# Linear attention and two expert stages on one core: a unit's outputs stand ahead of the next unit's state sum on TensorE

## The reference, cut to what matters

```python
gamma = 1.0 - 2.0 ** (-5.0 - np.arange(H))
for t in range(S):                      # B, H, S, D = 4, 8, 768, 64
    state = gamma * state + k[:, :, t] (outer) v[:, :, t]
    y[:, :, t] = scale * (q[:, :, t] @ state)
x = y.transpose(0, 2, 1, 3).reshape(3072, 512)
x = moe(x)        # argmax of x @ w_gate picks one of 8 experts, two products, two gates
return mlp(x)     # RMS norm, gate and value products, sigmoid, output product
```

## Time and profile before

| what | value |
|---|---|
| median of 3 executions | 1095.88 us (1095.04 to 1097.04) |
| the profiled execution: its time, its span | 1094.34 us, 1092.6 us |
| PE busy (matmuls) over the span | 1078.5 us (99%) |
| PE's weight loads, DVE, ACT, POOL busy | 82%, 42%, 35%, 17% |
| granted TensorE clock over the span | 1.00 of 2.4 GHz |

### The profile page before, as it was taken

The page is one execution under the profiler, slowest core; times in us unless marked ns, Lnnn a source line. Parts: engine busy times, 40 slices in busy tenths (PEclk is TensorE's granted clock), DMA queues, the critical chain, the costliest instruction groups (busy, mean ns, idle before and its releaser), DMA issues.

```text
span 1092.6 us, 20224 instructions
## 1 busy us (share of the span) xinstructions
PE 1078.5 (99%) x6195; PEld 895.1 (82%) x6196; DVE 454.7 (42%) x926; ACT 385.0 (35%) x619; POOL 186.5 (17%) x246
## 2 busy tenths in 40 slices
PE   7999999999999999999999999999999999999998
PEld 6888887888888888888888888888888888888887
DVE  4887766342414425333434232522433242333222
ACT  3554435443535555443232131322133131313112
POOL 3555514322321210000100300300030011001000
PEclk9999999999999999999999999999999999999999
DMA  9999635443445434433201210101020011101001
GB/s 221 256 254 266 168 128 203 153 116 125 125 116 189 167 115 137 147 105 112 70 6 34 78 38 2 65 12 38 0 77 21 17 38 38 38 0 39 1 1 38
DMA packets 114836, 102.57 MB, mean 94 GB/s; under 512 B 82112, under 2 KB 87648, under 8 KB 114784
## 3 DMA queue, kind: packets, MB, share of 16 engines
q1 hardware_dynamic: 99520, 67.12, 23.2%
q0 software_dynamic: 8832, 26.81, 7.4%
q10 hardware_dynamic: 6432, 7.96, 2.1%
HBM read 76.41 MB, written 20.22 MB: 88 GB/s over the span
## 4 chain that ended last, share of the span: by engine, by line
PE 94%; DVE 2%; DMA 1%; issue 1%; ACT 0%; SPq 0%; DVEq 0%; ACTq 0%; POOL 0%
PE bank L723 15%; PE bank L725 15%; PE bank L724 15%; PE banks L654 14%; PE bank L624 13%; PE banks L723 3%; PE banks L725 3%; PE banks L724 3%; PE banks L571 2%; PE banks L530 2%; PE bank L544 2%; PE bank L635 1%; PE banks L523 1%; PE banks L635 1%; PE bank L613 1%; PE bank L560 1%
## 5 line engine op out<-in xcount | busy, mean ns | idle before, releaser
L1424 DVE TENSOR_TENSOR gated<-bank,sig 128x512 f32<-128x512 f32 (+1 forms) x78 | 50.7, 649 | 312.3 <-ACT sig L1033 309.2
L1033 ACT ACTIVATE sig<-bank 128x512 f32<-128x512 f32 x72 | 43.1, 598 | 319.9 <-PE bank L725 306.7
L723 PE MATMUL bank<-xh,w1h 128*128 128x512 f32 x384 | 149.4, 389 | 0.0
L724 PE MATMUL bank<-xl,w1h 128*128 128x512 f32 x384 | 149.4, 389 | 0.0
L725 PE MATMUL bank<-xh,w1l 128*128 128x512 f32 x384 | 149.4, 389 | 0.0
L1042 ACT ACTIVATE hh<-prod 128x512 fp32r<-128x512 f32 (+1 forms) x78 | 46.7, 599 | 110.6 <-DVE prod L1432 106.1
L725 PEld LDWEIGHTS bank<-xh,w1l 128*128 128x128 f32 x384 | 72.1, 188 | 15.0
L724 PEld LDWEIGHTS bank<-xl,w1h 128*128 128x128 f32 x384 | 72.1, 188 | 15.0
L723 PEld LDWEIGHTS bank<-xh,w1h 128*128 128x128 f32 x384 | 72.1, 188 | 14.9
L1640 POOL DMA_INDIRECT out_rows<-x_out,cur_idx x10 | 10.1, 1010 | 407.9 <-ACT x_out L1049 318.7
L1438 DVE TENSOR_TENSOR hl<-prod,hh 128x512 fp32r<-128x512 f32 (+1 forms) x78 | 50.8, 651 | 51.5 <-ACT hh L1042 50.1
(11 more groups left out here) (241 smaller groups left out, 2073.0 us busy)
## 6 DMA issues: line engine op xcount, KB each, us to landing
stage<-in_moe_w SPq DMA_DIRECT2D x64, 512.0 KB
expert_rows<-tile_o ACTq DMA_DIRECT2D x29, 256.0 KB
q_raw<-in_q SPq DMA_DIRECT2D x24, 256.0 KB
k_raw<-in_k SPq DMA_DIRECT2D x24, 256.0 KB, 6.5
v_raw<-in_v SPq DMA_DIRECT2D x24, 256.0 KB
stage<-stage SPq DMA_DIRECT2D x80, 64.0 KB, 2.0
stage<-in_moe_w_out SPq DMA_DIRECT2D x6, 512.0 KB
stage<-in_moe_w_gate SPq DMA_DIRECT2D x5, 512.0 KB
```

The source lines that it names most:

```text
L723: pe.matmul(out_ap, lh, rh, start=first, stop=False, skip_group_check=True)
L724: pe.matmul(out_ap, lh, rl, start=False, stop=False, skip_group_check=True)
L1033: nc.scalar.activation(sig[:], bank[GV[f % 2][0]][:, :], ACT.Sigmoid).then_inc(s["sig_done"], 1)
L1424: v3.tensor_tensor(gated[:, part], bank[GV[f % 2][0]][:, part], sig[:, part], ALU.mult)\
```

## The change

In TensorE's `step(u)`, `outputs(u - 1)` is called ahead of `state_sum(u)`. Nothing else differs; the instructions of the other four engines stand in the same order as before.

```diff
@@ -588,9 +588,9 @@
 
             def step(u):
                 turn_qk(u)
-                state_sum(u)
                 if u:
                     outputs(u - 1)
+                state_sum(u)
                 if u == 2:
                     pe.wait_ge(s["mats_set"], 4)
                 if u > 1:
```

## The result

The change makes the kernel slower. Its median is 1099.38 us (7 executions) beside 1096.41 us of the kernel before (7 executions), a ratio of 1.0034 with a 95% interval of 1.0024 to 1.0044. On 1096 us this is +3.7 us (2.6 to 4.8); the forecast was +3.1.

What follows compares the result with a forecast made beforehand. TensorE was taken to set the time everywhere. 13 x 0.20, 3 x 0.32 and 0.2, less 0.65, made +3.1 us, on 1095.88 forecast as 1099.0 us; range 1097.0 to 1101.2.

Steps and rivals of the forecast that it cites:

- The mechanism: In TensorE's attention steps, the state sum fills the wait for the logits chain; moving it lays that wait bare.
- Steps with c = 0, 2, 3, 4: Attention steps with carried outputs and a state sum: +0.20 us each, the state sum taking 0.46 behind the outputs.
- Rival 1: The moved state sum costs its full 0.61 us: +2.8 over the forecast sum, 1101.8 us; 8 in 100.
- Steps with c = 1: Attention steps 7, 13 and 19, with no block of other shape between: +0.32 us each, the whole logits wait new.
- step 11: Attention step without a state sum, read before the change: outputs start 1.41 us behind its first transpose, after a bare wait.
- Steps 1 and 2: First attention steps with outputs: outputs fill the state sum's 1.33 us wait for v, giving back 0.65 us.
- Step 18 and late scatters: Attention step where TensorE already waits: a late scatter now costs all its lateness, +0 to +0.3, taken as 0.2 us.
- Rival 3: Behind the attention, 130 to 180 us: up to about 1.8 us of the delay is absorbed, 1097.3 us; 13 in 100.
- Rival 4: Joining two blocks of one tile shape removes a 0.15 us switch, if outputs start right behind the transposes: 1093.1 us; 5 in 100.

Runs made afterwards that it cites:

- e5: The changed kernel with VectorE summing the logits twice, released after the second sum; ratio 1.0086 to the kernel before.
- e6: The kernel before, old order kept, with VectorE summing the logits twice; ratio 1.0031 to the kernel before.
- e1: The kernel before with outputs ahead of the state sum only from step 3 on, steps 1 and 2 in the old order; ratio 1.0036.
- e9: The changed kernel timed once more, in a second set of executions; ratio 1.0034 to the kernel before.
- e7: The kernel before, old order kept, with masked scores times v ahead of the carried-state products inside the outputs; ratio 0.9986.
- e3: The changed kernel with the outputs' two waits swapped, the state copy waited for ahead of the logits; ratio 1.0017 to the kernel before.

## Why the prediction was right

- **The mechanism** held in every step: the logits chain releases the outputs in steps 2 to 23 (the forecast had 17 to 20 of them), and e5 against e6 shows that the state sum had covered it.
- **Steps with c = 0, 2, 3, 4** were forecast at +0.20 us and are +0.20 (5.72 against 5.52). The state sum costs 0.46 behind the outputs, as read from the block of the same shape. Rival 1, 0.61, is refuted. So is what I drew from the Trainium skill's rule on weight loads ("TensorE: Matmul & The Clock Gate", "What overlaps and what doesn't"): the state sum's weight loads follow the outputs' without a gap.
- **Steps with c = 1** were mis-sized: 0.24 instead of 0.32. I took +1.41 over from step 11, which has a second wait queued behind the logits; with one wait it is +1.30. That is -0.24 us in sum.
- **Steps 1 and 2**: the term of -0.65 us measured -0.15 in the profiled pair, and nothing in e1 against the full change. It took one execution's early first step as given, while the old order's wait for v absorbs a late step 1 and the new order doesn't.
- **Step 18 and late scatters**: the term was 0.2. In the pair, steps 12 and 14 were 0.09 and 0.37 late instead, and step 18 took 5.72 as it had taken 5.71. (Step 12's x_out was on time; what held its outputs for 0.09 us is open, and e9's step 12 has the same 0.09.) Between steps 3 and 23 the pair shows 111.35 - 107.54 = +3.8 us: 13 x 0.20, 3 x 0.24 and 0.46 late. The forecast for that stretch was 2.6 + 0.96 + 0.2 = 3.8. The errors in the terms, -0.24 and +0.26, cancelled by luck. At step 23 the pair's shift is 3.66 us where the forecast sum was 3.1, because steps 1 and 2 gave back 0.5 less. The measured 3.7 us (2.6 to 4.8) can't tell these two sums apart; it is the steps' lengths that bear the mechanism out.
- **Rival 3** fell: the shift of 3.66 us at step 23 goes through the stretch up to 350 us within 0.1 us, as read from ScalarE's line 876. Of the profiled pair's further +0.9 us, 0.8 comes in one pause of ScalarE at 370 us (below), and no other profile of the new order has a tail so long.
- **Rival 4** had its price right and its condition not met; e7 is what it looks like when the condition is.

## What to carry to other kernels

A block of matmuls that waits for nothing is worth most right ahead of the one whose release comes latest. Before moving it, measure how far its successor starts behind its release: the step without the block, if the kernel has one, shows the bare wait. Put blocks of one tile shape side by side where no wait lies between, and queue the wait that is satisfied last behind all others. A gain at the program's start that rests on when a load lands should be read from more than one execution.

## What the runs showed of the hardware

- A wait that is already satisfied, queued on TensorE behind the one that is waited for, costs 0.11 us after the release (0.46 against 0.35 us, in all steps of e3).
- TensorE's switch from one tile shape to another costs 0.15 to 0.17 us in fp32, and none stands between groups of 128*64 and 128*64. Between the state sum and the ranks (128*128) the idle weight load isn't shown, but the group's distance is 0.67 instead of 0.46 and holds it.
- Two pauses stay unexplained. ScalarE's line 876 starts 0.97 us behind the start of the product group ahead of it in the kernel before (366.20 - 365.23) and 1.79 us in the changed kernel's first profile (370.73 - 368.94):

```profile
370.73 0.60 ACT L876 ACTIVATE hid<-bank 128x512 f32<-128x512 f32 x1 [1.73 <-remote]
```

  TensorE stopped in step 11 of e3 in the middle of a group of products, where no wait is queued, and the step took 6.55 us instead of 5.15:

```profile
69.71 0.20 PEld L524 LDWEIGHTS banks<-qT,state 64*64 64x64 f32 x7 [1.36 <-issue]
```
